# Retention and two MLP layers on one core: table in three loads, other slots and banks in a span's first quad, layer 2's first weights ahead of x, p3's operand on DVE

## The reference

```python
for t in range(S):
    state = gamma * state + einsum('bhd,bhe->bhde', k[:, :, t], v[:, :, t])
    y[:, :, t] = scale * einsum('bhd,bhde->bhe', q[:, :, t], state)
x = y as rows (3072, 512)
h = x @ w_in;  x = (h * cos(h)) @ w_out                      # layer 1, d_ff = 2048
h = x @ w_in;  g = where(h >= 1, h, where(h <= -1, 0, (h + 1)**2 / 4))
out = g @ w_out                                              # layer 2
```

## Time and profile before

| what | value |
|---|---|
| median of three runs | 1102.44 us (1101.61 to 1102.63) |
| the profiled execution | 1101.37 us, its span 1099.6 us |
| PE busy | 1077.3 us, 98% |
| PE weight loads busy | 888.7 us, 81% |
| DVE, ACT, POOL busy | 681.1, 517.9, 242.2 us |
| granted clock of PE over the span | 0.995 of full |
| slices under full clock | the first of 40 (27.5 us): 0.8 |

### The profile page before, as it was taken

How to read it: one execution, slowest core, us unless ns; L and a number is a source line. 1 busy time by engine, 2 the same in 40 slices (tenths; PEclk the granted TensorE clock), 3 DMA queues, 4 the chain that set the end, 5 groups by cost and what they waited for, 6 DMA issues and landing times.

```text
span 1099.6 us, 14473 instructions
## 1 busy us (share of the span) xinstructions
PE 1077.3 (98%) x5572; PEld 888.7 (81%) x5572; DVE 681.1 (62%) x1021; ACT 517.9 (47%) x846; POOL 242.2 (22%) x278
## 2 busy tenths in 40 slices
PE   7899999999999999999998999999999999999998
PEld 5788888778888888888886888888888888888887
DVE  4777674566666545666658666656666646666632
ACT  5687763236656423666654454443323343323332
POOL 3977722330000122000116577500000000000000
PEclk8999999999999999999999999999999999999999
DMA  9355554424223442323252544550333350423111
GB/s 339 127 208 210 193 195 148 144 77 162 99 113 134 153 135 86 135 107 133 87 182 87 211 172 172 180 212 11 121 119 134 134 182 1 148 99 128 67 39 39
DMA packets 44452, 149.12 MB, mean 136 GB/s; under 512 B 4704, under 2 KB 4832, under 8 KB 42336
## 3 DMA queue, kind: packets, MB, share of 16 engines
q1 hardware_dynamic: 44384, 148.20, 37.8%
HBM read 106.24 MB, written 41.94 MB: 135 GB/s over the span
## 4 chain that ended last, share of the span: by engine, by line
PE 86%; DVE 4%; DMA 3%; POOL 3%; ACT 2%; SPq 1%; issue 1%; DVEq 0%; ACTq 0%; POOLq 0%
PE bank L520 13%; PE bank L524 13%; PE bank L522 13%; PE bank L554 8%; PE bank L555 8%; PE bank L553 8%; PE bank L549 7%; PE bank L550 6%; PE bank L551 6%; DMA kn_sb<-in_k_n 2%; PE bank L429 2%; POOL q_sb L1140 1%; DVE g_lo L769 1%; POOL kn_sb L1148 1%; DVE x_lo L702 1%; PE bank L456 1%
## 5 line engine op out<-in xcount | busy, mean ns | idle before, releaser
L520 PE MATMUL bank<-x_hi,tw 128*128 128x512 f32 x672 | 262.4, 390 | 3.8 <-DVE work L795 2.3
L524 PE MATMUL bank<-x_hi,tw 128*128 128x512 f32 x672 | 262.2, 390 | 0.0
L522 PE MATMUL bank<-x_lo,tw 128*128 128x512 f32 x672 | 262.0, 390 | 0.0
L549 PE MATMUL bank<-g_hi,wd_hi 128*128 128x512 f32 x384 | 152.7, 398 | 4.4 <-DVE g_lo L769 4.4
L520 PEld LDWEIGHTS bank<-x_hi,tw 128*128 128x128 f32 x672 | 126.6, 188 | 31.5 <-issue 4.9
L550 PE MATMUL bank<-g_lo,wd_hi 128*128 128x512 f32 x384 | 149.7, 390 | 0.0
L551 PE MATMUL bank<-g_hi,wd_lo 128*128 128x512 f32 x384 | 149.6, 390 | 0.0
L553 PE MATMUL bank<-wd_hi,g_hi 128*128 128x512 f32 x384 | 149.4, 389 | 0.0
L554 PE MATMUL bank<-wd_lo,g_hi 128*128 128x512 f32 x384 | 149.4, 389 | 0.0
L555 PE MATMUL bank<-wd_hi,g_lo 128*128 128x512 f32 x384 | 149.4, 389 | 0.0
L524 PEld LDWEIGHTS bank<-x_hi,tw 128*128 128x128 f32 x672 | 126.5, 188 | 26.4
(11 more groups left out here) (94 smaller groups left out, 1409.9 us busy)
## 6 DMA issues: line engine op xcount, KB each, us to landing
tw<-t_scratch SPq DMA_DIRECT2D x64, 896.0 KB, 6.4
t_scratch<-tw SPq DMA_DIRECT2D x16, 1792.0 KB, 7.5
work<-x_scratch SPq DMA_DIRECT2D x24, 256.0 KB, 3.6
raw<-in_w1u SPq DMA_DIRECT2D x16, 256.0 KB, 3.3
wd_raw<-in_w1d SPq DMA_DIRECT2D x8, 512.0 KB, 8.8
q_sb<-in_q_t SPq DMA_DIRECT2D x16, 256.0 KB, 2.7
k_sb<-in_k_t SPq DMA_DIRECT2D x16, 256.0 KB, 3.4
v_sb<-in_v_n SPq DMA_DIRECT2D x16, 256.0 KB, 3.1
```

The costliest lines, as they stand in the source:

```text
L520: nc.tensor.matmul(to[:, :], w[:, kt, 0, i, :], x_hi[:, i, kt, :], start=opens, stop=False, skip_group_check=True)
L522: nc.tensor.matmul(to[:, :], w[:, kt, 0, i, :], x_lo[:, i, kt, :], start=False, stop=False, skip_group_check=True)
L524: last = nc.tensor.matmul(to[:, :], w[:, kt, 1, i, :], x_hi[:, i, kt, :], start=False, stop=kt == 1, skip_group_check=True)
L549: nc.tensor.matmul(to[i][:, :], wd_hi[:, f, cols], g_hi[:, slot, :], start=opens, stop=False)
```

## The change

On SP, the table that was loaded in two pieces is loaded in three; the first pieces now hold the decay of q for units 0 and 1, then the small tables, then the rest. The raw weights of quad 0 are issued behind k of unit 4, ahead of q of unit 6; those of quad 1 ahead of the down weights. On ACT, the `scale_k` of the first units stand one by one behind the hi parts of x. On POOL, the first weights' sums come ahead of the scaling of q for units 6 and 7, in transitions q of the next unit comes ahead of k of this one, and p3's operand is gone: DVE makes it, in spans 0, 1 and 2. In a span's first quad other slots and banks are used: `sum_u3` writes slot 7 (`A21`) and `sum_h22` slot 6 (`H21`), p4 has a bank that p6 used, so that it waits for `sum_u2` and no longer for `sum_u3`, and p6 waits for the bank of y. In that quad `gate_low` stands ahead of the second `angle`. At the layer switch the hi parts of the first weights stand ahead of the copies of x, and the work on x stands two downs later.

```diff
-S1, U2, U3, H22, A22, A11, H21, A21, H12, A12 = range(10)
+S1, U2, U3, A22, A11, H21, A21, H12, A12 = 0, 1, 2, 4, 5, 6, 7, 8, 9
...
-SUMS_LATE = {3: [("s3", 0), ("s3", 1)], 4: [("s2", 0), ("s1", 0)], 5: [("s4", 0)], ...
+SUMS_LATE = {5: [("s3", 0), ("s3", 1)], 6: [("s2", 0), ("s1", 0)], 7: [("s4", 0)], ...
-HIGHS_LATE = {0: [("p1", 0), ("p1", 1)], 1: [("p2", 0), ("p2", 1)], 4: [("p7", 0), ("p7", 1)], ...
+HIGHS_LATE = {2: [("p1", 0), ("p1", 1)], 3: [("p2", 0), ("p2", 1)], 6: [("p7", 0), ("p7", 1)], ...
-LOWS_LATE = {1: [("p1", 0), ("p1", 1)], 2: [("p2", 0), ("p2", 1)], 4: [("p7", 0)], ...
+LOWS_LATE = {3: [("p1", 0), ("p1", 1)], 4: [("p2", 0), ("p2", 1)], 6: [("p7", 0)], ...
-MADE_LATE = [2, 3, 9, 10]
...
-            order = ((0, 3, 2, 1), (0, 3, 1, 2), (0, 2, 3, 1), (0, 1, 2, 3))[q if q < 1 else (q - 1) % 3 + 1]
+            order = ((0, 2, 3, 1), (0, 1, 2, 3), (0, 3, 1, 2))[q % 3]
...
-            sp.dma_start(tb[:, 0:P], table[:, 0:P]).then_inc(table_first, 16)
+            sp.dma_start(tb[:, 0:2 * P], table[:, 0:2 * P]).then_inc(table_first, 16)
             load_q(0)
             load_k(0)
-            sp.dma_start(tb[:, P:TABLE_WIDTH], table[:, P:TABLE_WIDTH]).then_inc(table_in, 16)
             load_q(1)
             load_k(1)
+            sp.dma_start(tb[:, small], table[:, small]).then_inc(table_in, 16)
             load_v(0)
             load_kn(0)
+            sp.dma_start(tb[:, 2 * P:KT * P], table[:, 2 * P:KT * P]).then_inc(table_rest, 16)
             for u in range(2, AHEAD):
                 load_q(u)
                 load_k(u)
                 load_v(u - 1)
                 load_kn(u - 1)
-            load_weights(0)
+                if u == 5:
+                    load_weights(0)
             load_v(AHEAD - 1)
             load_kn(AHEAD - 1)
+            load_weights(1)
             load_wd(0, 0)
...
                     if name == "p6" and s < PAIRS:
+                        y_taken(AHEAD * (s + 1) - 1 - (s == 0))
+                    if name == "p5" and s < PAIRS:
                         state_taken(AHEAD * (s + 1) - 1 - (s == 0))
-                    if name == "p5" and s < PAIRS:
-                        y_taken(AHEAD * (s + 1) - 1 - (s == 0))
...
                 if name == "p4":
-                    pe.wait_ge(u3_done, n + 1)
+                    if q == 0:
+                        pe.wait_ge(u2_done, n + 1)
+                    else:
+                        pe.wait_ge(u3_done, n + 1)
...
+            def x3_sum(s, kt):
+                dve.wait_ge(x_copied, COPIES * s + 2 + kt + 1)
+                dve.wait_ge(summed, NSUM * s + SUM_PLACE["s2", kt] + 1)
+                nc.vector.tensor_tensor(work[:, X12 + kt, :], work[:, X12 + kt, :], work[:, SUM2 + kt, :],
+                                        ALU.subtract).then_inc(x3_summed, 1)
...
                     x_sum(s, "s1", kt)
-                    if s == 0:
-                        update_state(AHEAD - 2)
+                    x3_sum(s, kt)
                     split_low(s, "p6", kt)
                     if lows:
                         gate_low(s - 1, *lows.pop(0))
                     split_low(s, "p5", kt)
+                    if s == 0:
+                        update_state(AHEAD - 2)
                     split_low(s, "p4", kt)
+                    split_low(s, "p3", 0)
                     for item in lows:
                         gate_low(s - 1, *item)
+                    split_low(s, "p3", 1)
...
                 if q == 0:
                     gate(s, q, 0)
+                    gate_low(s, 1, q)
                 angle(s, q, 1)
-                gate_low(s, 1, q)
+                if q:
+                    gate_low(s, 1, q)
...
-            for u in range(3):
-                scale_k(u)
+            scale_k(0)
             for u in range(AHEAD):
                 operands(0, u)
-                if u + 3 < AHEAD:
-                    scale_k(u + 3)
+                if u < 6:
+                    scale_k(u + 1)
                 if u < KT:
                     copy_state(u)
-                if u in (4, 5):
-                    t_high(u - 4)
-            t_high(2)
+                if u == 5:
+                    scale_k(7)
+                if u in (3, 4, 5):
+                    t_high(u - 3)
             t_high(3)
...
+                if s == PAIRS - 1:
+                    t_high(weight_item(QUADS * PAIRS, 0))
+                    t_high(weight_item(QUADS * PAIRS, 1))
...
-                            if n in MADE_LATE:
-                                t_high(weight_item(QUADS * PAIRS, 0) + MADE_LATE.index(n))
-                            if n == len(tail) - 1:
+                            if n in (1, 2):
+                                t_high(weight_item(QUADS * PAIRS + 1, n - 1))
+                            if n == 3:
                                 wd_high(1, 0)
...
-            def x3_operand(s):
...
-            pool.wait_ge(table_in, 16)
-            for u in range(3, AHEAD):
+            pool.wait_ge(table_rest, 16)
+            for u in range(3, 6):
                 scale_q(u)
-            for i in range(2):
-                t_sums(i)
-            for i in range(2):
-                t_low(i)
-            for i in range(2, 4):
-                t_sums(i)
-            x3_operand(0)
-            for i in range(2, 4):
-                t_low(i)
+            t_sums(0)
+            t_sums(1)
+            scale_q(6)
+            scale_q(7)
+            t_low(0)
+            t_low(1)
+            t_sums(2)
+            t_sums(3)
+            t_low(2)
+            t_low(3)
...
-                    for i in range(AHEAD):
+                    pool.wait_ge(table_in, 16)
+                    scale_q(u)
+                    for i in range(1, AHEAD):
                         scale_q(u + i)
-                        scale_k(u + i)
-                    x3_operand(s + 1)
+                        scale_k(u + i - 1)
+                    scale_k(u + AHEAD - 1)
```

65 lines of the change are left out of this document (35 added, 30 removed).

## The result

The changed kernel took **1092.49 us** (median of 4 runs, 1092.07 to 1093.48), the kernel before 1102.03 beside it (4 runs, 1101.35 to 1102.63): ratio **0.9915 [0.9898, 0.9932]**, 9.5 us sooner. The forecast was 1092.1, in 1088.5 to 1096.5. The profiled execution of after is the slowest of its four (1093.48, span 1091.7; the other spans are 1090.3, 1091.1 and 1090.3), so its first 60 us are read with care.

What follows compares the result with a forecast made beforehand. PE, busy 98% of the span, was taken as the bound, with about 18 us of lost time. Gains of 2.1 + 5.2 + 3.0 = 10.3 us gave a median of 1092.1 us, range 1090 to 1094, with neighbours 1088.5 to 1096.5.

Steps and rivals of the forecast that it cites:

- Part 3: Transitions: nine waits of scores for POOL's q go, 4.9 us; p3's operand on DVE 0.6; less 0.3; 5.2 us won.
- The charge of 0.3 for `gate_low`: Spans 1 and 2: `gate_low` ahead of the second `angle` delays a held down of quad 1 by 0.15 us each.
- Part 2: Span 0's first quad: first product to first down 2.6 us shorter, less 0.5 for the second down; 2.1 us won.
- Part 4: Layer switch: earlier weights' hi parts remove waits of downs for g_lo, 3.5 us, less 0.5 left; 3.0 us won.
- the gain of only 0.5: Layer switch: with the port pair an exclusive lock, Part 4 would be near 0.5 us and not 3.0.
- Part 1: Ahead of span 0: the 2.61 us wait goes, unit 6's scores wait some 3 us; nothing won by the first product.
- the clock's price: Ahead of span 0: slow clock behind unit 6's wait of 3 us charged at 1.4 us, as behind that of 2.61.
- The sum of 15.2 us: Span 0, first product to first down: 12.3 us of matmuls plus 2.9 of waits, if the clock stays up.
- The charge of 0.5 for the second down: Span 0, quad 1: the second down comes in reach of the curve's chain; 0.5 us charged.
- Rival "slower, DVE is the bound in itself": First spans: x's two-operand instructions slow in themselves, each moved one costs 1.7 us on PE's path; 1112 us, chance 0.02.
- Rival "the switch keeps its waits": Layer switch: POOL's work only moves to where x's work is and DVE pays there; 1094.6 us, chance 0.08.
- Rival "the start gives all": Ahead of span 0: the clock does not drop; 1089.4 us, chance 0.11.

Runs made afterwards that it cites:

- the experiment with the copy behind x: Against the changed kernel with q of unit 6 ahead of the raw weights: ACT's hi part of quad 1's first weights moved behind unit 6's x hi parts; 1090.77 us.
- the kernel whose p4 waits longer: The changed kernel with p4 of a span's first quad waiting for `sum_u3` again, as before the change; 1092.13 us.
- the seven kernels with after's quad in the table: Variants of the changed kernel: start order undone, PE kept busy, k before q, switch undone, unit 6's q first, plus copy moved, plus earlier switch; 1089.28 to 1097.71 us.

## Why the prediction was right, and where it was not

**Part 3, transitions: right in mechanism, a little more in size.** 5.2 forecast: 4.9 for the order of q and k, 0.6 for p3's operand, less 0.3. In the transitions 4.3 + 1.4 = 5.7 were won: 4.9 by the order, as the experiment that puts it alone into before shows (3.5 and 1.4 in the traces; 5.2 in the times), and 0.8 by the operand, as putting it back shows. The wait of 0.50 went, because DVE's last rows run at 0.68 with POOL idle. The charge of 0.3 for `gate_low` ahead of `angle` was wrong: the held downs of spans 1 and 2 wait 0.41 and 0.40 as they did. The smaller 3.35 + 1.32 = 4.7 of the landmark table has the 0.9 lost in span 0 in it, which belongs to Part 2.

**Part 4, switch: right.** 3.0 forecast with 0.5 left; 2.8 by the landmarks, the same 2.8 in the trace with it undone, 2.2 in the times. The one wait left, 1.24 and not 0.5, lies at 576.76, in before's time (5.1 us later) at the end of the stretch of 576 to 581 that the forecast named, and for its reason: DVE's rows beside POOL's last lo parts and `wd_lo` (3.20 for two and 1.76 for the g_lo). The forecast weighed a rule of the Trainium skill ("SBUF — State Buffer", "SBUF: two separate sides": one engine's use of the shared ports blocks the other). The traces bear that rule out better than the prediction said. In the experiment with the copy behind x, DVE's two and POOL's two together took from 37.24 to 40.73, 3.5 us; alone they take 1.29 (44.00 in after) and 2.27 (566.29 in after, DVE idle until the start of one g_lo), 3.6 in sum. At 46 us of after it is 3.3 against 3.6. What was wrong was the gain of only 0.5 that I drew from the rule for Part 4: it counted every instruction of x as blocked, and only those that met POOL's were, two lo parts and a g_lo in full.

**Part 1, start: its effect right, one term not fixed.** Unit 6's scores at 26.86, and undoing the order costs 0.5: worth nothing, as said. But the clock's price in the profiled execution was 13.54 - 10.68 = 2.9 us and not 1.4, so the first product came at 40.40 where 37.6 + 1.4 was forecast. In the kernel whose p4 waits longer the same clock price was 1.4 (26.61 to 38.68, 12.07 us), and with k ahead of q it was nothing. That it falls at all is not fixed by the wait: it fell after one of 3.05 and not after one of 2.95, and in before's start after 2.61 in one execution and not after 2.87 in another. What decides it was not tried. The Trainium skill ("TensorE: Matmul & The Clock Gate", "Part 1: The HAM clock gate") says that the chip's look at the activity isn't aligned to the program, so that one kernel's slow stretch differs from run to run; the two executions agree with that, and no run here shows the cause.

**Part 2, first quad: the first down about where forecast, by a wrong picture and some luck.** The forecast put the first down at 57.5 - 2.6 = 54.9; the seven kernels with after's quad in the table have 54.43 to 55.31. But the 57.49 that it started from held 1.5 us of slow clock. With before's start and quad and the clock up it is 55.92; from first product to first down that is 17.1 us, and 16.7 with the old start and the new quad. So at equal clock the quad itself gave 0.4, and Parts 1 and 2 together about 1.0 at the transition's first scores (173.15 to 172.0 to 172.2), where 2.1 were forecast. The sum of 15.2 us for the stretch had the matmuls and 2.9 of waits in it; after has 16.65, with 3.4 of waits and 1.0 of restarts, which the forecast left out. It also added PE's time from the first product to four small waits, as if an earlier product were an earlier down. It is DVE's chain that sets it: p6's wait, forecast 0.5, is whatever PE has won before (0.7, 2.1, 2.2, 3.95). The forecast took DVE's moved instructions at 0.6 each; two of them, at 46.70, took 2.55 beside POOL. The operand's move, which I let pass inside p4's and p3's waits, costs 1.6 to 2.2 us at the first down of span 0 and gains 0.8 at the end of the first transition; as a whole it is worth nothing (1091.99 against 1092.49), and with POOL in span 0 and DVE in the others 0.8 is won. How much of the quad's gain each of the other slots, banks and orders gave was not tried apart, except p4's wait, which is no term of its own. The charge of 0.5 for the second down was 0.9 in after's trace, most of it one product later, at 71.42.

**The sum.** By the profiled pair 7.9 us of 10.3, by the medians 9.5. The two differ because after's profiled execution is 1.0 above its median, by its slow start, and before's 0.7 below the median beside it. The 9.5 are 5.7 for the transitions and 2.8 for the switch by the traces, which leaves 1.0 for the start and the first quad. Against 5.2, 3.0 and 2.1 the errors are +0.5, -0.2 and -1.1: that the time lies 0.4 from the forecast is in part luck. Rival "slower, DVE is the bound in itself" fell: 0.68 us at 232 to 236 for all four kinds. Rival "the switch keeps its waits" fell. Rival "the start gives all" did not come, and would not have with the clock up, because the clock was not what held the first down.

## What to carry to other kernels

On an engine that serves several others in order, put first what is waited for first: swapping two scalings gave 5 us here for no work less. Ahead of removing a wait, follow the queue to the one behind it: 4.9 us of an earlier first product were worth 0.5 in the time, since another wait of the same stage ended last. Compare stages at an equal clock: 1.5 us of what the first quad seemed to offer was a slow stretch of one execution. One placement of an operand need not be right for all stages: in span 0, where POOL is busy and slows DVE's rows (2.55 for two), p3's operand was better on POOL, and at the end of the first transition, where POOL is otherwise idle (0.68 a row on DVE), on DVE.
